# Attention, routed experts and a Mish MLP in one kernel: a reordered start, a joined hand-over, moved weight pieces and end steps

## The reference

```python
# attention: q, k, v (2, 8, 1152, 64)
q_pool = q.reshape(B, H, S // 2, 2, D).mean(axis=3)
attn = softmax(q_pool @ k.T / sqrt(D)); x = attn @ v      # 1152 rows of 512
# routed experts: 8 experts, w1 512x1024, w2 1024x512
e = argmax(x @ w_gate); gain = softmax(x @ w_gate)[e] * sigmoid(x @ w_output_gate)[e]
x = gain * (relu(x @ w1[e]) @ w2[e])
# MLP: w_in 512x2048, w_out 2048x512
h = x @ w_in; out = (h * tanh(softplus(h))) @ w_out
```

## Time and profile before

| | |
|---|---|
| median of 3 runs | 702.13 us |
| profiled execution | 705.92 us, span 704.0 us |
| PE busy | 679.1 us (96%) |
| DVE busy | 507.6 us (72%) |
| ACT busy | 406.8 us (58%) |
| POOL busy | 80.9 us (11%) |
| attention, until | 293 us |
| hand-over, until | 311.5 us |
| experts, until | 492.5 us |

### The profile page before, as it was taken

How to read it: one execution, slowest core, us unless ns; L and a number is a source line. 1 busy time by engine, 2 the same in 40 slices (tenths; PEclk the granted TensorE clock), 3 DMA queues, 4 the chain that set the end, 5 groups by cost and what they waited for, 6 DMA issues and landing times.

```text
span 704.0 us, 14844 instructions
## 1 busy us (share of the span) xinstructions
PE 679.1 (96%) x5198; PEld 598.3 (85%) x5198; DVE 507.6 (72%) x1193; ACT 406.8 (58%) x819; POOL 80.9 (11%) x115
## 2 busy tenths in 40 slices
PE   6999999999999999979999999999999999999996
PEld 5888888888888888679989989998889988899994
DVE  5667677768677767576566666666999988787873
ACT  4656575666565666515655566576666655454542
POOL 3302131404040300040000000000000000001001
PEclk9899999999999999989999999999999999999999
DMA  7667979797969520079990464041300000001001
GB/s 188 149 197 215 266 221 255 178 260 179 247 159 238 120 52 2 1 278 379 399 348 18 150 238 151 15 135 30 121 1 0 1 1 1 10 36 46 0 1 45
DMA packets 91095, 93.83 MB, mean 133 GB/s; under 512 B 41248, under 2 KB 65824, under 8 KB 90528
## 3 DMA queue, kind: packets, MB, share of 16 engines
q1 hardware_dynamic: 87280, 84.39, 41.4%
q10 hardware_dynamic: 2320, 4.00, 1.9%
q0 software_dynamic: 1440, 4.72, 1.7%
HBM read 59.80 MB, written 16.78 MB: 109 GB/s over the span
## 4 chain that ended last, share of the span: by engine, by line
PE 86%; DVE 8%; ACT 2%; issue 2%; DMA 1%; POOL 0%; SPq 0%; ACTq 0%; DVEq 0%
PE score_banks L1037 14%; PE turn L815 12%; PE score_banks L1066 11%; PE pvT L796 11%; PE score_banks L1051 10%; PE score_banks L772 5%; PE score_banks L773 5%; PE score_banks L1088 4%; PE turn L1088 4%; PE pvT L1088 4%; PE turn L736 1%; PE turn L1015 1%; DMA raw_k<-k 1%; PE turn L1024 1%; DVE numer L1610 1%
## 5 line engine op out<-in xcount | busy, mean ns | idle before, releaser
L815 PE MATMUL turn<-ident,prob 128*128 128x128 f32 x648 | 111.5, 282 | 3.9 <-DVE x_tok L1395 1.4
L1342 DVE TENSOR_REDUCE nmax_part<-score_banks 128x1 f32<-128x768 f32 x72 | 68.9, 957 | 60.5 <-PE score_banks L773 47.1
L1037 PEld LDWEIGHTS score_banks<-xsT,w_slot 128*128 128x128 f32 x832 | 97.5, 196 | 5.0 <-issue 4.0
L1037 PE MATMUL score_banks<-xsT,w_slot 128*128 x832 | 97.8, 280 | 3.8 <-DVEq L1560 3.8
L815 PEld LDWEIGHTS turn<-ident,prob 128*128 128x128 f32 x648 | 77.5, 142 | 26.1 <-issue 13.8
L1134 ACT ACTIVATE prob<-score_banks,nmax 128x1152 f32<-128x1152 f32 x72 | 87.5, 1215 | 1.6 <-DVE nmax L1352 1.5
L1141 ACT ACTIVATE probT<-turn 128x384 f32<-128x384 f32 x72 | 35.4, 491 | 89.2 <-PE turn L815 89.1
L796 PE MATMUL pvT<-probT,v_sb 128*64 128x128 f32 (+1 forms) x1404 | 85.9, 269 | 0.0
L772 PE MATMUL score_banks<-kT,qT 128*128 128x384 f32 x192 | 80.0, 417 | 4.6 <-DVE qT L1371 3.9
L796 PEld LDWEIGHTS pvT<-probT,v_sb 128*64 128x64 f32 x1404 | 69.5, 137 | 11.9 <-issue 11.9
L1574 DVE TENSOR_TENSOR w_lo<-w_slot,w_hi 128x512 fp32r<-128x512 f32 x104 | 68.2, 687 | 3.1 <-ACT w_hi L1254 3.0
(11 more groups left out here) (237 smaller groups left out, 1374.9 us busy)
## 6 DMA issues: line engine op xcount, KB each, us to landing
w_slot<-moe_w SPq DMA_DIRECT2D x16, 2048.0 KB, 13.2
slots_dram<-zeros SPq DMA_DIRECT2D x8, 1472.0 KB, 11.3
raw_k<-k SPq DMA_DIRECT2D x16, 288.0 KB, 6.3
v_sb<-v SPq DMA_DIRECT2D x16, 288.0 KB, 4.3
w_in_sb<-moe_w_in SPq DMA_DIRECT2D x2, 2048.0 KB, 8.0
w_out_sb<-moe_w_out SPq DMA_DIRECT2D x2, 2048.0 KB, 9.5
kT<-k_hi SPq DMA_DIRECT2D x14, 288.0 KB, 4.3
kT<-k_lo SPq DMA_DIRECT2D x14, 288.0 KB, 5.1
```

The source lines that it names most:

```text
L815: last = pe.transpose(bank[:, j * P:(j + 1) * P], prob[:, s % 2, c * KC + j * P:c * KC + (j + 1) * P], ident[:, :])
L1037: last = pe.matmul(h1_bank[f % 4][:, 0:P], w1_e[:, d, f * P:(f + 1) * P], xsT[:, d, bass.ds((t % XS_RING) * P, P)], start=(d == 0), stop=( ...
L1342: dve.tensor_reduce(nmax_part[:, s, 0:1], scores[s % 2][:, lo:lo + 2, 0:KC], AX.XY, ALU.max, negate=True).then_inc(max_part, 1)
```

## The change

**Data and orders.** The pieces of `w_in` go three, three and one behind the experts and one in step 6. The scaled tokens get memory of their own. The units of the start are reordered.

```diff
-        first_pieces = {RING + 1: ((0, 0), (0, 1)), RING + 2: ((1, 0), (1, 1)), RING + 3: ((0, 2), (1, 2))}
-        late_pieces = {4: (0, 3), 6: (1, 3)}
-        PIECES_READY = (3, 4, 6, 8)
+        first_pieces = {RING + 1: ((0, 0), (0, 1), (0, 2)), RING + 2: ((1, 0), (1, 1), (0, 3)), RING + 3: ((1, 2),)}
+        late_pieces = {6: (1, 3)}
+        PIECES_READY = (4, 5, 7, 8)
...
+        x_early = sb("x_early", [P, EARLY, D], F32, ring_at[3] + X_EARLY_IN)
+        x_late = sb("x_late", [P, TPH - EARLY, D], F32, ring_at[3])
...
-        WARM_BEFORE, WARM_BETWEEN = 20, 8
+        WARM_BEFORE, WARM_BETWEEN, WARM_BEHIND = 20, 8, 12
...
-                       ("k", 1, 2, 3), ("q", 0, (FIRST_PAIR, FT), 4), ("k", 1, 0, 1), ("q", 0, (FT, Q0), 5),
-                       ("k", 1, 1, 2), ("q", 1, (0, FT), 4)]
-        FIRST_Q_READY, FIRST_BANK0_FREE, FIRST_PAIR_READY, FIRST_BANK1_FREE, FIRST_TURN_FREE = 4, 5, 6, 8, 9
+                       ("k", 1, 2, 3), ("q", 0, (FT, Q0), 5), ("k", 1, 0, 1), ("k", 1, 1, 2),
+                       ("q", 0, (FIRST_PAIR, FT), 4), ("q", 1, (0, FT), 4)]
+        FIRST_Q_READY, FIRST_BANK0_FREE, FIRST_BANK1_FREE, FIRST_TURN0_FREE, FIRST_TURN_FREE, FIRST_PAIR_READY = 4, 5, 6, 7, 8, 9
...
+        def x_out(t):
+            return x_early[:, t, :] if t < EARLY else x_late[:, t - EARLY, :]
```

```diff
-            firsts = {0: first_tile(0), 1: first_tile(1)}
+            firsts = {0: 0, 1: first_tile(1)}
...
-            sp.wait_ge(logits_turned, 2)
-            load_w1(2, 2)
...
-            load_w2(2, 2)
+            load_expert(2, 2)
...
-                if i < EARLY:
-                    pool.wait_ge(slots_ready, 1)
-                    pool.wait_ge(early_x_scaled, i + 1)
-                else:
-                    pool.wait_ge(slots_ready, 2)
-                    pool.wait_ge(x_scaled, i - EARLY + 1)
+                pool.wait_ge(slots_ready, 1 if i < EARLY else 2)
+                pool.wait_ge(x_scaled, i + 1)
...
-                                        x_tok[:, i, :], None).then_inc(xs_stored, 16)
+                                        x_out(i), None).then_inc(xs_stored, 16)
```

```diff
-                    if not (first and s == 0):
+                    if first and s == 0:
+                        pe.wait_ge(first_ready, FIRST_TURN0_FREE)
+                    else:
...
-                            if i2 == FIRST_PAIR:
-                                pe.wait_ge(first_ready, FIRST_PAIR_READY)
-                            elif i2 == FT:
+                            if i2 == FT:
...
-                        qk((s + 2) % SB, 0)
+                        if not (first and s == 0):
+                            qk((s + 2) % SB, 0)
...
+                        if first and s == 0:
+                            pe.wait_ge(first_ready, FIRST_PAIR_READY)
+                            qk(2, 0)
...
-            def place_first(t):
+            def place_first(t, parts):
...
-                if t < EARLY:
-                    pe.wait_ge(early_x_scaled, t + 1)
-                else:
-                    pe.wait_ge(x_scaled, t - EARLY + 1)
-                for d in range(DT):
+                for d in parts:
...
+            place_first(0, (0, 2))
...
-            place_first(0)
+            place_first(0, (1, 3))
+            place_first(1, range(DT))
...
-            for t in range(1, TPH):
-                last = place_first(t)
+            for t in range(2, TPH):
+                last = place_first(t, range(DT))
...
+            keep_warm(WARM_BEHIND // 2, pvT)
+            for cols in (192, 256):
+                for m in range(3):
+                    pe.matmul(pvT[:, 0:cols], qT[:, 1, 1, 0:P], qT[:, 1, 1, P:P + cols], start=True, stop=True)
...
-                pe.wait_ge(stage_landed, 16 * t + 16)
-                pe.wait_ge(xs_copied, t + FILL_AHEAD)
-                fill_xs(t + FILL_AHEAD, fill_bank[0], stage)
...
+                    if f == FILL_AT:
+                        pe.wait_ge(stage_landed, 16 * t + 16)
+                        pe.wait_ge(xs_copied, t + FILL_AHEAD)
+                        fill_xs(t + FILL_AHEAD, fill_bank[0], stage)
...
-                for n in range(TC):
+                for n in range(TC - 1):
...
-                    if n == 0:
-                        pe.wait_ge(g_lo_ready, FT2 * CHUNKS)
+                pe.wait_ge(g_lo_ready, FT2 * CHUNKS)
+                for n in range(TC - 1):
...
+                product(FT2 - 2, TC - 1)
+                product(FT2 - 1, TC - 1).then_inc(y2_tile_done, 1)
```

```diff
+            def scale(t):
+                act.activation(x_out(t), x_tok[:, t, :], ACT.Copy, scale=gain[:, t:t + 1]).then_inc(x_scaled, 1)
...
+            act.wait_ge(gain_ready, 1)
+            scale(0)
...
-            act.wait_ge(early_gain_ready, 1)
-            scale_early(0)
+            scale(1)
...
-            scale_early(1)
+            scale(2)
...
-            for t in range(2, EARLY):
-                scale_early(t)
+            scale(3)
...
+            act.wait_ge(gain_ready, 2)
+            for t in range(EARLY, TPH):
+                scale(t)
...
+            act.wait_ge(y1_copied, 1)
...
-                copy_xs(t + FILL_AHEAD, fill_bank[0], (t + FILL_AHEAD) % XS_RING)
...
+                    if f == W2_RING + FILL_AT:
+                        copy_xs(t + FILL_AHEAD, fill_bank[0], (t + FILL_AHEAD) % XS_RING)
...
-                    if f:
+                    if first and f <= 1:
+                        if f == 0:
+                            g_high(c, 0, True)
+                    elif f:
...
-                    elif not first:
+                    else:
```

```diff
+                invert_sums(k, it)
+                take_o(k, it)
+            def invert_sums(k, it):
...
-                dve.wait_ge(pv_done, done + 1)
+            def take_o(k, it):
+                dve.wait_ge(pv_done, GB * it + k + 1)
...
-                    if first and s == 0:
-                        first_low(LATE_UNIT)
+                    if first and s < 2:
+                        first_low(FIRST_PAIR_READY - 1 + s)
...
-                        end_group(k, it)
+                        invert_sums(k, it)
+                    pick(0)
+                    invert_gain(0)
+                    for k in (GB - 2, GB - 1):
+                        take_o(k, it)
...
-            def gain_inverse(n):
+            def invert_gain(n):
...
+                dve.reciprocal(gain[:, tiles], gain_inv[:, tiles]).then_inc(gain_ready, 1)
...
-                dve.tensor_scalar(onehot[:, t, :], slot_iota[:, :], slot_f[:, t:t + 1], None, ALU.is_equal
-                                  ).then_inc(onehot_ready, 1)
+                dve.tensor_scalar(onehot[:, t, :], slot_iota[:, :], slot_f[:, t:t + 1], gain[:, t:t + 1],
+                                  ALU.is_equal, ALU.mult).then_inc(onehot_ready, 1)
...
-            for n in range(FIRST_BANK0_FREE):
+            for n in range(FIRST_BANK1_FREE):
...
-            for n in range(FIRST_BANK0_FREE, FIRST_BANK1_FREE):
+            max_first(1, 1)
+            for n in range(FIRST_BANK1_FREE, FIRST_TURN_FREE):
...
-            max_first(1, 1)
-            first_low(FIRST_TURN_FREE - 1)
...
-            pick(0)
-            gain_inverse(0)
-            dve.reciprocal(gain[:, 0:EARLY], gain_inv[:, 0:EARLY]).then_inc(early_gain_ready, 1)
...
+            dve.wait_ge(gain_ready, 1)
...
+            invert_gain(1)
...
-            gain_inverse(1)
-            then(dve.reciprocal(gain[:, EARLY:], gain_inv[:, EARLY:]))
+            dve.wait_ge(gain_ready, 2)
...
-                dve.tensor_scalar(x_tok[:, t, :], x_tok[:, t, :], gain[:, t:t + 1], None, ALU.mult
-                                  ).then_inc(x_scaled, 1)
...
+            dve.sem_inc(h1_ready, 4)
...
-            dve.sem_inc(h1_ready, 4)
```

```diff
-            def mlp_chunk(c, first):
+            def mlp_chunk(c, first, final):
...
-                    if f >= 2:
+                    before = (c, f - 1) if f else (c - 1, FT2 - 1)
+                    if first and f == 0:
+                        mish_prod(c, f)
+                        mish_ratio(c, f)
+                        mish_gated(c, f)
+                    elif first and f == 1:
+                        g_low(c, 0)
+                        mish_prod(c, f)
+                    elif final and f == FT2 - 1:
+                        mish_ratio(*before)
...
-                    elif not first:
-                        g_low(c - 1, FT2 - 2 + f)
-                    before = (c, f - 1) if f else (c - 1, FT2 - 1)
-                    if first and not f:
+                        mish_gated(*before)
...
+                        if f > 2 or not first:
+                            g_low(*((c, f - 2) if f >= 2 else (c - 1, FT2 - 2 + f)))
...
-                mlp_chunk(c, c == 0)
+                mlp_chunk(c, c == 0, c == CHUNKS - 1)
+            mish_ratio(CHUNKS - 1, FT2 - 1)
...
-            mish_ratio(CHUNKS - 1, FT2 - 1)
```

18 lines of the change are left out of this document (9 added, 9 removed).

## The result

The changed kernel takes 695.38 us (median of four runs, 694.61 to 695.75), beside 702.36 for the kernel before in the same comparison: ratio 0.9895, 95% interval 0.9878 to 0.9912. The difference of the medians is 7.0 us; the ratio gives 7.4. I forecast 691.0 with a range of 688.0 to 696.5: the direction and the range hold, and the gain was over-stated by 4 us. From profile to profile it is 10.2 us (705.92 to 695.75), near the 11.1 that I had summed. Why these two differences are 3 us apart is the question that most of the experiments serve.

What follows compares the result with a forecast made beforehand. PE, 86% of the chain, was taken to bound the kernel through its idle times and lower clock. Terms -3.3 - 6.6 - 1.0 + 1.6 - 1.1 - 0.7 = -11.1 gave 694.8 us profiled, 691.0 as median; range 688.0 to 696.5.

Steps and rivals of the forecast that it cites:

- Hand-over: From attention into the first expert: PE starts 3.6 us earlier and the clock holds, saving 2.95; together -6.6 us.
- Loop: Expert tile loop: `x2_high` ahead of the stage copy splits ACT's fifth weight block 0.5 us earlier; -1.0 us, bounds 0 and -1.8.
- Pieces: Input pieces: a third one behind experts 5 and 6 makes PE stand 0.8 us each time; +1.6 us, bounds 0 and 2.4.
- MLP: MLP block 0: first product ready earlier and one late piece gone; -1.1 us, bounds -0.4 and -1.4.
- End: Last MLP steps: `g_lo(15)` ends earlier, POOL issues its three scatters 1.27 apart; -0.7 us, bounds -0.5 and -1.3.
- the start, "-3.3 us": First scores: reordered units and full clock bring the first `pv` to 23.3 to 23.8 instead of 27.04; bounds -1.0 and -3.8.
- a clock of 0.50 at either place: Sign of being wrong: granted clock at half rate at the start or behind the first expert matmul; no size given.
- the start gives little: Rival at the first scores: work mostly changes its order and the clock can fall; price 2.3 us, 693.3, chance 0.12.
- I take differences from the profile and set them against the median: Whole kernel: savings read from the 705.92 us profiled execution are subtracted from the 702.13 median, 3.79 below.
- The clock fell at the new hand-over: Rival at the first expert: the clock falls there anyway; price 2.95 us, 694.0, chance 0.2.
- The gap did not move into the first tile: Rival at the first expert tile: the gap moves there as a wait for stage or ACT; up to 2.0 us, chance 0.08.
- The weights of expert 2: Slower rival: PE waits for expert 2's late weights; price 12.5 us or more, 703.5 and up, chance 0.03.

Runs made afterwards that it cites:

- more_warm_up: The changed kernel with 28 instead of 20 transposes before the keys land and 14 instead of 8 before the first scores; 700.32 us, ratio 0.9933.

## Why the prediction was right, and where it was not

**From the last `pv` on it was right.** To the end the span leaves 411.8, 411.8 and 411.0 us in the three profiles of before and 404.0 in the changed kernel: 7.0 to 7.9 less. The forecast for these parts was -6.6 - 1.0 + 1.6 - 1.1 - 0.7 = -7.8. The sum is closer than its terms: the loop gave 0.9 more than forecast, the pieces took up to 0.6 more and the MLP gave 0.3 less, and these errors offset each other.

- *Hand-over*, forecast -6.6: the way from the last `pv` to the expert is 3.9 to 4.2 us shorter (15.4 for 19.4 to 19.6), and the 64 matmuls are 2.7, 2.5 and 1.4 faster by the three profiles of before. So 5.6 to 6.6. The mechanism (start behind the placement, clock held) was right, and the price of the clock was the largest of three. What the filler was meant to do it did not have to do. All that I called hidden was hidden: marks with two operands took 1.37 us for five (step 0.26, between my bounds), the late scalings 3.17 for five on ACT, the first `hT_lo` ended at 308.69, and the stage had about 2.8 us to spare.
- *Loop*, forecast -1.0: -1.9, just beyond the bound. *Pieces*, forecast +1.6: +1.6 as PE's wait, and 2.2 as the stretch.
- *MLP*, forecast -1.1: -0.8 (MLP and end are 1.4 to 1.5 shorter, 0.7 of it the end's); the late piece gives 1.2 and block 0 at once takes 0.4 back. *End*, forecast -0.7: -0.7, with POOL's scatters 1.27 apart as said.

**The step that failed is the start, "-3.3 us".** It took the clock of 0.50 in the earlier trace rows for a property of the old order and let "steps 0 and 1 at full clock" follow from the new one. In four profiles of the old order the clock held once, and in ten of the new one it never did through the whole stretch; the 2.06 us before the first exponential is the idle time that is left. The prediction had named "a clock of 0.50 at either place" as a sign of being wrong, and it stood at 0.50 from 17.4 to 20.0; the first `pv` was not below 24.5 and the gap in the scores not gone. Of the 2.3 us between the two profiled executions at the first `pv`, about 1.2 is the order, and how much of that reaches the last `pv` is not told apart from nothing. The rival "the start gives little" named the clock, at 2.3 us dearer than the forecast; it was the likelier case, and I gave it 0.12.

**The sentence "I take differences from the profile and set them against the median" failed with it.** The profiled execution lay 3.8 us above a median of three runs that was itself 1.4 to 2.3 below the later medians. Two other profiles of before have spans of 700.9 and 700.7; against them the changed kernel's 693.9 is 6.9 less, as the medians say. Of the 3.1 us between the first and the second profile 2.0 lie ahead of the first `pv`, where only the first had a half-speed stretch, and about 1 within attention, unexplained. A gain that removes what makes one execution slow can't be taken in full from a median that doesn't have it. That profile to profile came out at 10.2, near the 11.1, was in part luck: the one execution drew the long half-speed stretch at the start and the other the short one.

**The rivals.** The clock fell at the new hand-over in one profile of eleven. The gap did not move into the first tile. The weights of expert 2 were no wait in any. Time lost inside the joined stretch did appear, but in no list of mine: the stall of 3.7 us inside the placement, in all four profiles of one set, on one chip.

**Open.** What PE lacks in that stall: that each of its lines says "issue" would fit the supply of instructions, but no run shows it, and the DMA queues carry the same two instruction packets around the placement with the stall (298.46 and 305.63) as without (295.17 and 302.50 in the changed kernel). Nor is it known whether the kernel before has it on that chip; there its wait of 3.8 us would hide it, and its median of 704.38 beside 703.51 and 703.93 elsewhere would fit, but it was not profiled there. Whether the scatters cause it was not settled either: in all four profiles the stall ends 0.1 to 0.2 us before the last packet of the late scatters, but both stand at a fixed distance from the placement, so this may be chance, and on the other chips the same scatters ran without a stall. No run undoes the whole hand-over alone, so its two parts, the earlier start and the held clock, are read from the stretches. Not tried: the pieces two, two, three with the old block 0.

## What to carry to other kernels

Ask of the profiled execution how it stands to the median before taking any difference from it: if it lies 3.8 us above, take more runs and a second profile first, find what the one has that the other lacks (here a half-speed stretch), and count that part of the gain as chance. A stage may be shortened by 1.2 us at its start without anything to be seen of it at its end; a stretch between marks that the edit doesn't touch, compared over several profiles, tells this better than one pair. Where a wait is removed, what used to lie inside it is exposed; here that may be a stall that one chip showed and two others did not.

## What the runs showed of the hardware

- The same kernel with the same 3.1 us of idle time on PE had a granted clock of 0.50 around and behind it for the whole 5.8 us from 17.40 to 23.20 in one execution, for a shorter time in another (0.83 in the mean from 15 to 25 us, against 0.66), and never in a third (1.00). At the hand-over it fell with 3.8 us of idle time in three of three, and did not with 2.50 in the one profile that has it, while at the start it fell with 2.06 to 2.9, in all ten profiles of the new order. The length of the idle time alone does not decide.
- Transposes alone raised PE's rate: in more_warm_up the step of the first 28, with nothing run before them, went from 0.21 to 0.11 us at 4.4 us.
- PE lost 3.7 us in straight-line code with nothing that the profile shows it waiting for: one or two matmuls every 0.71 us, for the last seven to nine of the placement, in four of four profiles on one chip and in none of the ten others.
